# Windowed attention in front of two MLPs: mask, row maximum and value product done another way

## What is computed

```python
scores = scale * np.matmul(q, k.transpose(0, 1, 3, 2))          # scale = 1/8
mask = (rel >= 0) & (rel < window)                              # window = 64
attn = softmax(np.where(mask, scores, -1e9))                    # divided by (sum + 1e-9)
x = (attn @ v) laid out as (2304, 512)
xn = x / np.sqrt(np.mean(x * x, -1, keepdims=True) + 1e-6) * rms_g
h = silu(xn @ w_gate) * (xn @ w_val)                            # d_ff 1536
x2 = h @ w_out
h2 = x2 @ w_in
out = (h2 * sigmoid(1.702 * h2)) @ w_out2                       # d_ff 2048
```

## Time and profile before

| | us |
|---|---|
| median of 3 runs | 964.01 |
| lowest, highest | 963.85, 965.39 |
| the profiled execution, its own time | 963.56 |
| its span, first to last instruction | 961.8 |
| TensorE busy | 940.5 (98%) |
| TensorE weight loads busy | 797.3 (83%) |
| VectorE busy | 405.6 (42%) |
| ScalarE busy | 359.8 (37%) |
| GpSimd busy | 103.8 (11%) |

### The profile page before, as it was taken

The page is one execution under the profiler, slowest core; times in us unless marked ns, Lnnn a source line. Parts: engine busy times, 40 slices in busy tenths (PEclk is TensorE's granted clock), DMA queues, the critical chain, the costliest instruction groups (busy, mean ns, idle before and its releaser), DMA issues.

```text
span 961.8 us, 12297 instructions
## 1 busy us (share of the span) xinstructions
PE 940.5 (98%) x4728; PEld 797.3 (83%) x4756; DVE 405.6 (42%) x740; ACT 359.8 (37%) x751; POOL 103.8 (11%) x145
## 2 busy tenths in 40 slices
PE   6699999999999999999999999999999999999998
PEld 5699888888888888888888888888888888888897
DVE  4798544434444344443444462233223222422332
ACT  3576565534555335553211132222223222322232
POOL 3465101010010100101012220000000000000000
PEclk9999999999999999999999999999999999999999
DMA  6565122201112011210312231002002000200000
GB/s 209 180 213 185 34 66 68 75 24 57 61 60 76 22 62 58 64 34 1 132 36 104 81 130 45 1 0 88 1 1 88 1 1 0 66 1 1 11 35 22
DMA packets 33419, 57.56 MB, mean 60 GB/s; under 512 B 3408, under 2 KB 9040, under 8 KB 33360
## 3 DMA queue, kind: packets, MB, share of 16 engines
q1 hardware_dynamic: 32496, 55.49, 17.8%
q10 hardware_dynamic: 864, 1.28, 0.4%
HBM read 47.32 MB, written 9.44 MB: 59 GB/s over the span
## 4 chain that ended last, share of the span: by engine, by line
PE 96%; DVE 2%; ACT 1%; POOL 1%; issue 0%; DMA 0%; DVEq 0%; POOLq 0%
PE ps L496 23%; PE ps L498 22%; PE ps L497 22%; PE ps L596 7%; PE ps L597 7%; PE ps L598 7%; PE ps L447 3%; PE ps L479 3%; PE ps L467 2%; DVE w_all L794 1%; PE ps L486 0%; DMA kwin<-in_k_t 0%; DVE probT L772 0%; POOL sq L394 0%; PE ps L456 0%
## 5 line engine op out<-in xcount | busy, mean ns | idle before, releaser
L496 PE MATMUL ps<-x_hi,w_all 128*128 128x512 f32 (+1 forms) x800 | 304.5, 381 | 4.5 <-DVE x_lo L785 4.1
L498 PE MATMUL ps<-x_lo,w_all 128*128 128x512 f32 (+1 forms) x800 | 295.2, 369 | 0.0
L497 PE MATMUL ps<-x_hi,w_all 128*128 128x512 f32 (+1 forms) x800 | 295.0, 369 | 0.0
L496 PEld LDWEIGHTS ps<-x_hi,w_all 128*128 128x128 f32 x800 | 151.4, 189 | 29.4 <-issue 4.4
L498 PEld LDWEIGHTS ps<-x_lo,w_all 128*128 128x128 f32 x800 | 151.3, 189 | 25.9
L497 PEld LDWEIGHTS ps<-x_hi,w_all 128*128 128x128 f32 x800 | 151.6, 190 | 24.8
L898 DVE TENSOR_TENSOR hid<-ps,sig 128x512 f32<-128x512 f32 (+1 forms) x80 | 51.1, 638 | 207.6 <-ACT sig L710 207.4
L710 ACT ACTIVATE sig<-ps 128x512 f32<-128x512 f32 (+1 forms) x80 | 44.5, 556 | 215.4 <-PE ps L498 215.4
L596 PE MATMUL ps<-w_all,h_hi 128*128 128x512 f32 x288 | 112.2, 390 | 0.0
L597 PE MATMUL ps<-w_all,h_hi 128*128 128x512 f32 x288 | 112.2, 390 | 0.0
L598 PE MATMUL ps<-w_all,h_lo 128*128 128x512 f32 x288 | 112.0, 389 | 0.0
(11 more groups left out here) (91 smaller groups left out, 975.8 us busy)
## 6 DMA issues: line engine op xcount, KB each, us to landing
wstage<-in_w_a SPq DMA_DIRECT2D x36, 256.0 KB, 3.1
qbd<-in_q_bd SPq DMA_DIRECT2D x35, 256.0 KB, 2.7
vwin<-in_v_win SPq DMA_DIRECT2D x33, 256.0 KB, 2.8
wstage<-in_w_b SPq DMA_DIRECT2D x32, 256.0 KB, 3.1
kwin<-in_k_t SPq DMA_DIRECT2D x33, 160.0 KB, 2.9
out_dram<-late SPq DMA_DIRECT2D x18, 256.0 KB, 2.5
xT<-x_scratch SPq DMA_DIRECT2D x4, 1024.0 KB, 5.2
x_scratch<-wstage SPq DMA_DIRECT2D x3, 1024.0 KB, 4.2
```

The costliest lines, as they stand in the source:

```text
L496: pe.matmul(out_, w[:, 0, cols], xh, start=first, stop=False)
L497: pe.matmul(out_, w[:, 1, cols], xh, start=False, stop=False)
L498: return pe.matmul(out_, w[:, 0, cols], xl, start=False, stop=last)
```

## The change

Three things change, with the order of the opening.

- **Mask.** The bf16 product, `both`, its waits and VectorE's copies of the mask are gone. `mask` is now two fp32 masks of 128 partitions, made by GpSimd in 8 selects. VectorE takes scores and mask block by block in one instruction, writes their masked, scaled and negated sum to `prob` and accumulates its minimum, the negated maximum. The exponentials read `prob` in place with scale -1. The wait of the exponentials for the transposes of two steps before moves to `row_max`, and `scores(s)` waits for the maximum of the step before instead of its exponentials.
- **Value product.** Each block's product is split into two of 64 columns of v and 64 columns of probabilities, each writing its 64 partitions, so that the 256 output columns of a step are dense. One copy of 128 partitions x 256 columns on ScalarE replaces the two half copies, in every step.
- **Opening.** On VectorE the reciprocals of steps 1 to 3 and the fourth maximum come ahead of copies of transposed probabilities; on GpSimd `normalise(2)` and `normalise(3)` move up by one place. `scale_x(0)` and the low parts of x are interleaved; the first low part of the weights stands ahead of the fourth copy.

```diff
-            both = sb("both", [P, P], BF16, at)
-            mask = sb("mask", [P, 2 * GB, P], BF16, at)
+            mask = sb("mask", [P, 2, P], F32, at)
...
+            for first in (1, 0):
+                for h in range(2):
+                    rows = slice(h * BLK, (h + 1) * BLK)
+                    then(nc.gpsimd.affine_select(out=mask[rows, first, :], in_=mask[rows, first, :],
+                                                 compare_op=ALU.is_ge, fill=NEG, base=BLK,
+                                                 pattern=[[-1, P]], channel_multiplier=1))
...
             normalise(0)
             normalise(1)
+            normalise(2)
             squares(0)
-            normalise(2)
+            normalise(3)
             squares(1)
-            normalise(3)
...
             def scores(s):
...
-                    wait(pe, exp_done, s)
+                    wait(pe, max_ready, s)
                     pe.wait_ge(qk_loaded[s % 2], 32 * ((s - EARLY) // 2 + 1))
                 for i in range(GB):
-                    pe.matmul(bank[:, i, :], q_of(s)[:, i * P:(i + 1) * P], k_of(s)[:, i * BLK:i * BLK + P],
-                              start=(i == 0), stop=False, skip_group_check=True)
...
-                pe.matmul(bank, both[:, :], mask[:, from_:from_ + GB, :], start=False, stop=True,
-                          skip_group_check=True).then_inc(scores_done, 1)
+                    ins = pe.matmul(bank[:, i, :], q_of(s)[:, i * P:(i + 1) * P], k_of(s)[:, i * BLK:i * BLK + P],
+                                    start=True, stop=True)
+                ins.then_inc(scores_done, 1)
...
                 for i in range(GB):
-                    ins = pe.matmul(ps[:, o_bank(s), i * P:(i + 1) * P], v_of(s)[:, i * P:(i + 1) * P],
-                                    probT_of(s)[:, i * P:(i + 1) * P], start=True, stop=True)
+                    for h in range(2):
+                        cols = slice(i * P + h * BLK, i * P + (h + 1) * BLK)
+                        ins = pe.matmul(ps[h * BLK:(h + 1) * BLK, o_bank(s), i * BLK:(i + 1) * BLK],
+                                        v_of(s)[:, cols], probT_of(s)[:, cols], start=True, stop=True)
                 ins.then_inc(pv_done, 1)
...
+            def evacuate_o(s):
+                t, c, at_ = home_of(s)
+                act.wait_ge(pv_done, s + 1)
+                wait(act, x_hi_ready, DC * t)
+                wait(act, x_lo_ready, DC * t)
+                nc.scalar.copy(xT[:, c, at_:at_ + GT], ps[:, o_bank(s), 0:GT]).then_inc(o_evacuated, 1)
+
             def exponentials(s):
                 act.wait_ge(max_ready, s + 1)
-                if s >= EARLY + 2:
-                    act.wait_ge(probs_transposed, s - 1)
                 for i in range(GB):
-                    ins = nc.scalar.activation(prob_block(s, i), ps[:, s_bank(s), i * P:(i + 1) * P],
-                                               ACT.Exp, bias=nmax[:, s % EARLY, i:i + 1], scale=float(HEAD) ** -0.5,
+                    ins = nc.scalar.activation(prob_block(s, i), prob_block(s, i),
+                                               ACT.Exp, bias=nmax[:, s % EARLY, i:i + 1], scale=-1.0,
                                                accum_out=rsum[:, s % EARLY, i:i + 1])
...
             def row_max(s):
...
-                nc.vector.tensor_reduce(peak, src, AX_X, ALU.max, negate=True).then_inc(max_order, 1)
-                dve.wait_ge(max_order, s + 1)
-                nc.vector.tensor_scalar(peak, peak, float(HEAD) ** -0.5, None, ALU.mult).then_inc(max_ready, 1)
+                if s >= EARLY + 2:
+                    dve.wait_ge(probs_transposed, s - 1)
+                if s == 0:
+                    dve.wait_ge(masks_made, 4)
+                for i in range(GB):
+                    batch_first = 1 if (GB * group + i) % PER_BATCH == 0 else 0
+                    ins = nc.vector.tensor_tensor_reduce(
+                        out=prob_block(s, i), in0=ps[:, s_bank(s), i * P:(i + 1) * P], in1=mask[:, batch_first, :],
+                        scale=-float(HEAD) ** -0.5, scalar=3.0e38, op0=ALU.add, op1=ALU.min,
+                        accum_out=nmax[:, s % EARLY, i:i + 1])
+                ins.then_inc(max_ready, 1)
...
             row_max(2)
-            evacuate_probT(0)
             reciprocal_of_sum(1)
             row_max(3)
+            evacuate_probT(0)
+            reciprocal_of_sum(2)
             evacuate_probT(1)
-            reciprocal_of_sum(2)
+            reciprocal_of_sum(3)
             evacuate_probT(2)
-            reciprocal_of_sum(3)
+            weights_lo_A(0, 0)
             evacuate_probT(3)
-            weights_lo_A(0, 0)
             weights_lo_A(0, 1)
-            scale_x(0)
+            dve.wait_ge(rinv_ready, 1)
+            scale_x(0, 0)
+            scale_x(0, 1)
             dve.wait_ge(g_loaded, 16)
-            split_x_lo(0, TILES_A[0][1], True)
+            for d in range(DC):
+                split_x_lo(0, d, TILES_A[0][1], True)
+                if d + 2 < DC:
+                    scale_x(0, d + 2)
...
                     hid_lo_A(t, c)
-                    if first <= s - 1 < last:
-                        evacuate_o(dve, nc.vector.tensor_copy, 0, s - 1)
```

More of the change, by code:

```diff
@@ L155, in fused_attention_mlps @@
         pv_done = sem("pv_done")
-        o_evacuated = [sem(f"o_evacuated{h}") for h in range(2)]
+        o_evacuated = sem("o_evacuated")
         squares_done = sem("squares_done")
@@ L348, in then @@
                 pool.wait_ge(pool_order, order[0])
-            rows = slice(0, BLK)
             pool.wait_ge(zeros_made, 1)
-            then(nc.gpsimd.affine_select(out=mask[rows, 2, :], in_=mask[rows, 2, :],
-                                         compare_op=ALU.is_ge, fill=NEG, base=BLK,
-                                         pattern=[[-1, P]], channel_multiplier=1))
-            nc.gpsimd.affine_select(out=mask[rows, 2, :], in_=mask[rows, 2, :],
-                                    compare_op=ALU.is_gt, fill=NEG, base=0,
-                                    pattern=[[1, P]], channel_multiplier=-1).then_inc(masks_made, 1)
@@ L358, in _ @@
-            then(nc.gpsimd.affine_select(out=mask[rows, 3, :], in_=mask[rows, 3, :],
-                                         compare_op=ALU.is_ge, fill=NEG, base=BLK,
-                                         pattern=[[-1, P]], channel_multiplier=1))
-            then(nc.gpsimd.affine_select(out=mask[rows, 3, :], in_=mask[rows, 3, :],
-                                         compare_op=ALU.is_ge, fill=NEG, base=-BLK,
-                                         pattern=[[1, P]], channel_multiplier=0))
@@ L364, in _ @@
[L364 to L367 removed]
+            for first in (1, 0):
[4 more added lines that the diff above has]
+                                                 pattern=[[-1, P]], channel_multiplier=1))
+                    if first:
+                        nc.gpsimd.affine_select(out=mask[rows, 1, :], in_=mask[rows, 1, :],
+                                                compare_op=ALU.is_ge, fill=NEG, base=-BLK,
+                                                pattern=[[1, P]], channel_multiplier=0).then_inc(masks_made, 1)
+                    else:
+                        nc.gpsimd.affine_select(out=mask[rows, 0, :], in_=mask[rows, 0, :],
+                                                compare_op=ALU.is_gt, fill=NEG, base=0,
+                                                pattern=[[1, P]], channel_multiplier=-1).then_inc(masks_made, 1)
@@ L463, in transpose_probs @@
                 else:
-                    for h in range(2):
-                        pe.wait_ge(o_evacuated[h], s)
+                    pe.wait_ge(o_evacuated, s)
                 for i in range(GB):
@@ L472, in probs_by_v @@
                     pe.wait_ge(v_early_loaded[s], 16)
-                    for h in range(2):
-                        wait(pe, o_evacuated[h], s - 1)
+                    wait(pe, o_evacuated, s - 1)
                 else:
@@ L652, in _ @@
             for s in range(EARLY):
-                for h in range(2):
-                    evacuate_o(act, nc.scalar.copy, h, s)
+                evacuate_o(s)
             inverse_rms(0)
@@ L872, in _ @@
                     if c == SUMSQ_AT and last:
-                        scale_x(t + 1)
+                        dve.wait_ge(rinv_ready, t + 2)
+                        for d in range(DC):
+                            scale_x(t + 1, d)
                     if t == NA - 1:
@@ L878, in _ @@
                 dve.wait_ge(val_done, CA * (t + 1))
-                if t + 1 < NA:
-                    split_x_lo(t + 1, TILES_A[t + 1][1], True)
-                else:
-                    split_x_lo(NA, TILES_B[0][1], False)
+                for d in range(DC):
+                    if t + 1 < NA:
+                        split_x_lo(t + 1, d, TILES_A[t + 1][1], True)
+                    else:
+                        split_x_lo(NA, d, TILES_B[0][1], False)
                 n = TILES_A[t][1]
```

(3 more changed lines are left out.)

75 lines of the change are left out of this document (19 added, 56 removed).

## The result

The changed kernel takes 955.1 us (median of 4 runs, 954.24 to 955.72) against 963.93 before (4 runs beside them): ratio 0.9909, 95% interval 0.9895 to 0.9922. The forecast was 957.4 in a range of 941 to 970. The total is close; where it came from is not what the forecast said.

A forecast was written before the change was run, and what follows sets the result against it. TensorE's instruction stream bounds the kernel past 50 us, a chain of waits through all engines before. Mask -6.6, halves +1.3, opening -1.3 sum to -6.6 us: 957.0 from the profiled 963.56, 957.4 as median; range 941 to 970.

The forecast's parts named there:

- The scores' distance: Sign past 100 us: the second matmul behind the scores starts 1.12 us after their first record instead of 1.34.
- behind the value product the distance: Sign past 100 us: first record to second matmul behind, 1.1 to 1.2 us; near 0.7 overlap, over 1.4 bare change.
- Part 1, mask product: TensorE's mask product removed: 0.22 us saved in each of 30 steps where TensorE is full, 6.6 us.
- Part 2, the maximum: Mask and maximum in four VectorE instructions: 1.1 us per step, covered by TensorE from 50 to 92 us.
- The rival of a slow instruction: VectorE's new instructions take 2.2 us per step, so no change, 964 to 965 us; chance 0.08.
- Part 3, the value product: TensorE's value product in halves: 0.93 us per step, 0.04 more, over 32 steps 1.3 us lost.
- I take the value nearest to the rows that exist: Choice for the halved value product between half the time (0.46 us) and bare width changes (loss of 0.35 to 0.70).
- the side by side rival: Two halves of a value product stream together, 0.46 us instead of 0.89; 941 us, half overlap 949; chance 0.20.
- the bare change: Rival: TensorE waits 0.35 us per step entering half width, perhaps again leaving; 968.6 us, twice 980; chance 0.23.
- Part 4, the opening: Opening reordered: steps 2 and 3 earlier by 0.9 us, one copy saved 0.4, together 1.3 us gained.
- 5.8, still under TensorE's new 6.5: covered: From 50 to 92 us VectorE's load per chunk falls from 6.0 to 5.8 us, below TensorE's 6.5, costing nothing.
- booking no gain for it: Opening: interleaving starts the first gate product about 0.8 us earlier, but VectorE ends as late; nothing booked.

The follow-up runs named there:

- e2: The changed kernel with the value product at full width and the two half output copies again; 959.2 us, ratio 0.9946.
- e6: The changed kernel with each value product in tiles 1 to 3 parted into two half-width visits around the projection's last quarter; 964.8 us, ratio 1.0012.
- e4: The changed kernel with all four products of half 0 before the four of half 1, so not in turn; 964.2 us, ratio 1.0006.
- e1: The kernel before with only the value product in halves and the single ScalarE output copy; 963.1 us, ratio 0.9988.
- e3: The changed kernel with the opening in its old order, GpSimd's normalisations and the scaling of x included; 956.6 us, ratio 0.9916.
- e5: The changed kernel with one of VectorE's three low weight parts in tile 0 moved into its wait for the exponentials; 948.5 us, ratio 0.9841.
- e8: The changed kernel with GpSimd's high weight parts ahead of the squares in tile 0; 955.0 us, ratio 0.9909.
- e10: The changed kernel with squares over 8 of 256 columns in 6 of 8 steps under tile 0, output wrong; 952.1 us, ratio 0.9883.
- e9: The changed kernel with a VectorE low weight part in the wait (e5) and GpSimd's high parts ahead of the squares (e8); 951.0 us, ratio 0.9864.

## Why the prediction was right, and where only its total was

The forecast time came close by luck: the terms were wrong by more than the total. By its own signs the forecast is half borne out. The scores' distance is 1.13 us as it said and VectorE's maximum 0.92; but behind the value product the distance is 0.95 (150.78 to 151.73), between the 1.1 to 1.2 of the forecast and the 0.7 of overlap, and TensorE is no longer full from 50 us on.

**Part 1, mask product, 0.22 us x 30.** Right in the price: 0.21 in order of time, 5.2 us over 24 steps in e2. Wrong in the count: the six steps in tile 0 from 50 us on gained nothing, as TensorE did not set the pace there.

**Part 2, the maximum.** Forecast 1.1 us per step, measured 0.84 until VectorE is free and 0.92 until the result (four starts 0.21 apart). The rival of a slow instruction (2.2 us) is out.

**Part 3, the value product.** Forecast 0.93, a loss of 1.3 us in all; measured 0.80, a gain of 2.0 to 2.3 in tiles 1 to 3. The step that failed is "I take the value nearest to the rows that exist", that is, neither rival. Both were true at once and nearly cancel: the side by side rival's 0.46 us come out of e6 as 0.45 (16 x 0.028), and the bare change was priced at 0.35 at entry and comes out as 0.28 for entry and exit together. That the net is close to the forecast's small number is luck. The Trainium skill (TensorEngine Tiling (Array Packing), Key Properties) has both rules, that tiles run in parallel and that a change of tiling mode drains the engine; e4 and e6 agree with them, with 0.018 us less per record in turn and 0.36 us fixed per visit, 0.28 more than at full width. The Trainium skill's rule in TensorE: Matmul & The Clock Gate, LDWEIGHTS, columns / 1.2 ns, gives an estimate of 0.85 us for 16 loads of 64 columns one after another. The trace does not agree: the 16 loads take 0.55 us, and all of them and their products start within 0.62 us, so the rule does not bound the step here.

**Part 4, the opening.** Forecast -1.3, measured -3.9 to the first MLP product and -2.45 to the first SiLU (e1: halves and single copy 1.7 to the first product; e3: the order up to 3.3, disturbed by the clock). Transposes of step 2 start at 16.59, forecast 17.35: the term that was too big is the value product, 0.69 us instead of 1.13, and two of them lie ahead of this point. The shorter maxima gained nothing there: the fourth scores did not start 0.43 earlier, as forecast, but at 10.44 (10.37 before), held by the load of k. From the start of the scaling of x to the first MLP product 1.0 us more is gained (3.07 before, 2.10 after), but not by the interleaving, as e3 in the old order has 1.97; the cause stays open. To the first SiLU the interleaving costs about half a microsecond (6.9 us from the start of the scaling, in e3 6.1, before 6.4), so booking no gain for it was right.

**Tile 0.** The step that failed outright: "5.8, still under TensorE's new 6.5: covered". The sum of VectorE's busy time is not its loop. Its chunk is a ring: SiLU, maximum, then 0.8 us of standing for ScalarE's exponentials, normalisation, low parts, next SiLU. Busy 5.8 plus 0.8 is 6.6, over the new 6.5 already, and the squares add up to 1 us. Even with the 0.65 us of wait that the kernel before has it would have been 6.45, with nothing to spare. The row for that wait was in the trace of before (VectorE's reciprocals waited 0.5 to 0.66 us for the exponentials in each chunk from 50 us on), and I didn't read it. Its SiLUs already stood 6.9 to 7.5 us apart there, not 6.73. I had also called VectorE's lost copy a pure gain; with it went the order in time in which GpSimd's square was stretched and not the low parts.

Measured against forecast, in profiled spans: mask and halves from the second mark on -7.5 (forecast -5.3 + 1.0 = -4.3), opening -3.9 (-1.3), tile 0 +2.8 (-1.0). Three errors of 2.6 to 3.8 us left 2.0 in the sum. With the first SiLU as the mark between the last two they are -2.45 and +1.3, and the errors 3.2, 1.2 and 2.3. So of tile 0's +2.8 half is the choice of the mark and about half the second fall of the clock (last section), while what mask and halves gain there, 0.3 us per chunk, is eaten by VectorE's longer loop.

## What to carry to other kernels

When an edit shortens the engine that sets the pace, check the others not by their busy share but by their ring: busy time plus the waits inside it, against the new period; and fill those waits first (in e5 that gave 6.6 us on top). Half-width products on TensorE are worth it in turn and in one visit per batch of work: 0.028 us per fp32 record of 64 columns against 0.36 us per visit, so that the four blocks of a step barely pay here. As an estimate from these numbers, a block saves 0.09 us (0.36 / 4), the change of shape costs 0.28, and three blocks would be even; no run has three. An engine relieved of a copy also loses the moment that copy set for its neighbours.

## What the runs showed of the hardware that I had not expected

**The half-width visit.** Of the 0.36 us the trace of after shows 0.08 ahead of the first record and 0.10 behind the last, 0.18 in all, and a load that starts with its product instead of ahead of it. The other half lies inside the 0.62 us in which the records start. Only e6 brought it out.

**VectorE and GpSimd.** A VectorE instruction with two SBUF inputs of 512 columns takes 0.68 us alone and up to 1.23 beside GpSimd's squares; in other chunks it is GpSimd's square, 0.61 us alone in the opening, that takes 2.2. In the two chunks shown VectorE's run starts first in both, 0.33 us ahead of the square where VectorE is stretched and 0.15 us ahead where the square is. No run isolates what decides it.

**The clock.** TensorE's granted clock in the kernel after was at half, 1.2 GHz, from 24.8 to 31.6 us and again from 45.3 to 48.7, in the kernel before only from 29.8 to 33.2. Around the first fall in either kernel TensorE waits 3 to 4 us for the first low part of x. The second fall followed a wait of 2.53 us for the copy of the transposed probabilities, with 256-column matmuls 0.21 us apart behind it instead of 0.12 (TensorE in order of time):

```profile
44.32 0.69 PE L453 MATMUL ps<-probT,vwin 128*64 128x64 f32 x16 [2.53 <-DVE probT L757]
44.94 0.38 PE L470 MATMUL ps<-x_hi,w_all 128*128 128x256 f32 x1
45.16 0.32 PE L471 MATMUL ps<-x_hi,w_all 128*128 128x256 f32 x1
45.28 0.41 PE L472 MATMUL ps<-x_lo,w_all 128*128 128x256 f32 x1
45.50 0.42 PE L470 MATMUL ps<-x_hi,w_all 128*128 128x256 f32 x1
45.71 0.41 PE L471 MATMUL ps<-x_hi,w_all 128*128 128x256 f32 x1
```

The wait alone does not explain the fall. e8 has the same wait, of 2.55 us, at the same place, and its clock stayed up, with the 256-column matmuls behind it at 0.12 (TensorE in order of time, then the stretch from 45 to 50 us of e8 and of after):

```profile
45.19 0.69 PE L453 MATMUL ps<-probT,vwin 128*64 128x64 f32 x16 [2.55 <-DVE probT L757]
```

```profile
45.00:50.00 5.00, 4.81 (x52) 4.77 (x53) 4.15 (x12) 4.31 (x10) 1.36 (x2) 1.00 0.67 194
```

```profile
45.00:50.00 5.00, 5.00 (x31) 5.00 (x31) 4.93 (x15) 3.54 (x5) 1.77 (x2) 0.66 0.60 181
```

e10 likewise waits 2.53 us there and keeps its clock, and e9 falls after a wait of 2.04. What decides it stays open. What it costs can be read: 10 matmuls of 0.09 more and scores of 1.41 instead of 0.80, about 1.5 us, and e8, without the fall, has a tile 0 that is 1.3 us shorter than after with low parts as slow. So about half of the 2.8 us is the clock's, where it falls a second time. e5, with a single fall (25.8 to 29.2), lost nothing there. The falls differ from run to run in the opening as well, which is why first products compare only to a microsecond.
